# Chunk 0's inverse with one operand in PSUM and GpSimd beside it, block-diagonal inverses in its solves, and chunk 1's grams ahead of them

## What is computed

```python
y[t]  = q[t] @ state
v_old = state.T @ k_n[t]
state = state + beta[t] * outer(k_n[t], v[t] - v_old)
```

## Time and profile before

| | |
|---|---|
| median of three runs | 999.22 us |
| the profiled execution's own time | 1000.15 us |
| its span in the profile | 998.2 us |
| TensorE's granted clock, mean over the span | 0.993 of 2.4 GHz |
| busy time: TensorE, VectorE, ScalarE, GpSimd | 981.7, 583.1, 419.2, 25.4 us |

### The profile page before, as it was taken

The page is one execution under the profiler, slowest core; times in us unless marked ns, Lnnn a source line. Parts: engine busy times, 40 slices in busy tenths (PEclk is TensorE's granted clock), DMA queues, the critical chain, the costliest instruction groups (busy, mean ns, idle before and its releaser), DMA issues.

```text
span 998.2 us, 24906 instructions
## 1 busy us (share of the span) xinstructions
PE 981.7 (98%) x10566; PEld 804.3 (81%) x10566; DVE 583.1 (58%) x1465; ACT 419.2 (42%) x749; POOL 25.4 (3%) x34
## 2 busy tenths in 40 slices
PE   6899999999999999999999999999999999999998
PEld 6578788888888888888888888888888888888887
DVE  7769878776877687769535774433434334334332
ACT  4777544433434434424445553333333233333332
POOL 2510000000000000000000000000000000000000
PEclk9889999999999999999999999999999999999999
DMA  6342232003200410020003411001010010000000
GB/s 217 97 160 72 69 97 77 10 18 94 76 10 18 114 56 18 18 65 33 2 12 128 158 64 64 1 1 64 0 64 1 1 64 1 27 6 1 32 1 32
DMA packets 28413, 50.97 MB, mean 51 GB/s; under 512 B 2320, under 2 KB 15760, under 8 KB 28304
## 3 DMA queue, kind: packets, MB, share of 16 engines
q1 hardware_dynamic: 28304, 49.39, 15.3%
HBM read 39.94 MB, written 9.44 MB: 49 GB/s over the span
## 4 chain that ended last, share of the span: by engine, by line
PE 96%; ACT 2%; issue 1%; DMA 1%; DVE 0%; SPq 0%; DVEq 0%; ACTq 0%
PE psum L1120 40%; PE psum L1096 39%; PE psum L903 3%; PE psum L880 2%; PE psum L972 2%; PE psum L920 2%; PE psum L856 1%; PE psum L1009 1%; PE psum L929 1%; PE psum L1017 1%; PE psum L1040 1%; PE psum L1004 1%; ACT ring L622 1%; PE psum L1013 0%; DMA kt_sb<-in_k_t 0%
## 5 line engine op out<-in xcount | busy, mean ns | idle before, releaser
L1120 PE MATMUL psum<-g_hi,w 128*128 128x512 f32 x1152 | 392.1, 395 | 0.1
L1096 PE MATMUL psum<-x_hi,w 128*128 128x512 f32 x1152 | 387.0, 390 | 0.0
L1382 DVE TENSOR_TENSOR g_lo<-act_g,g_hi 128x512 fp32r<-128x512 f32 x192 | 132.6, 691 | 214.5 <-ACT g_hi L746 214.3
L1120 PEld LDWEIGHTS psum<-g_hi,w 128*128 128x128 f32 x1152 | 216.1, 188 | 50.8 <-issue 2.0
L1096 PEld LDWEIGHTS psum<-x_hi,w 128*128 128x128 f32 x1152 | 216.2, 188 | 45.6 <-issue 0.2
L746 ACT ACTIVATE g_hi<-act_g 128x512 fp32r<-128x512 f32 x192 | 121.4, 632 | 273.3 <-PE psum L1120 239.4
L1120 PE MATMUL psum<-g_lo,w 128*128 128x512 f32 x576 | 224.6, 390 | 0.0
L1096 PE MATMUL psum<-x_lo,w 128*128 128x512 f32 x576 | 224.1, 389 | 0.0
L1376 DVE TENSOR_TENSOR act_g<-act_g 128x512 f32<-128x512 f32 x96 | 66.4, 692 | 112.9 <-ACT act_g L739 112.9
L1096 PEld LDWEIGHTS psum<-x_lo,w 128*128 128x128 f32 x576 | 108.1, 188 | 22.4 <-issue 0.2
L1120 PEld LDWEIGHTS psum<-g_lo,w 128*128 128x128 f32 x576 | 108.2, 188 | 20.6
(11 more groups left out here) (101 smaller groups left out, 607.5 us busy)
## 6 DMA issues: line engine op xcount, KB each, us to landing
kt_sb<-in_k_t SPq DMA_DIRECT2D x24, 256.0 KB, 4.0
qt_sb<-in_q_t SPq DMA_DIRECT2D x24, 256.0 KB, 3.6
kn_sb<-in_k_n SPq DMA_DIRECT2D x20, 256.0 KB, 4.1
ring<-in_v_s SPq DMA_DIRECT2D x24, 192.0 KB, 2.7
between_layers<-y_out SPq DMA_DIRECT2D x6, 768.0 KB, 5.1
x_sb<-between_layers SPq DMA_DIRECT2D x6, 768.0 KB, 5.7
result<-y_out SPq DMA_DIRECT2D x5, 768.0 KB, 3.9
wi_st<-in_w_in SPq DMA_DIRECT2D x7, 384.0 KB, 3.1
```

Source lines behind the costliest of these rows:

```text
L1096: ins = pe.matmul(h_ps[n % 2][:, :], w_in_part(layer, f // GW, part)[:, kt, fs], x[:, kt, :], start=(kt == 0 and j == 0), stop=(kt == KT - ...
L1120: ins = pe.matmul(acc[kt][:, :], w_out_part(layer, f // GW, part)[:, f % GW, ds], g[n % 2][:, :], start=(f == 0 and j == 0), stop=(f == NF ...
L1382: dve.tensor_tensor(g_lo[n % 2][:, :], act_g[n % 2][:, :], g_hi[n % 2][:, :].bitcast(F32), ALU.subtract).then_inc(g_lo_ready, 1)
```

## The change

It does the following.

1. VectorE's inverse of chunk 0 writes the scaled diagonal blocks into PSUM banks 0 and 1 (`diag_ps`) and the products of each step into bank 2, so that each of its instructions has at most one input in SBUF. `x_inv` stays in SBUF. The later chunks' inverses are as they were.
2. GpSimd no longer waits for `xc`. It clears a new tile `xc_bd`, scales the values of chunk 0 (four instructions, in place of ScalarE's 32), takes the low parts of groups 0 and 1, and masks; after `xc` it copies the inverses of blocks k = 1 to 3 into `xc_bd`, 12 copies, as block-diagonal 128x128 matrices, and then takes the low parts of groups 2 and 3 (group 3 was VectorE's).
3. `first_solve` for k = 1 to 3 uses one 128x128 matmul for a head where there were four of 32x32.
4. The grams of chunk 1, all four, are made before chunk 0's solves and go to a tile of their own, `gram1`. `gram1` and `xc_bd` lie where the weights of the last two groups come later, so ScalarE waits for `s_done` before it writes group 7.
5. Order: TensorE's `keep_busy` instructions start at j = 25, use bank 3, and are longer between the stages; ScalarE cuts groups 2 and 3 before the solves; SyncE issues group 2 ahead of group 3; VectorE starts chunk 1's inverse and does its first three steps before `x_low_first`.

```diff
+        xc_bd = ahead_of_last.enter_context(nc.sbuf_tensor("xc_bd", [P, (NB - 1) * H, P], F32))
+        gram1 = [ahead_of_last.enter_context(nc.sbuf_tensor(f"gram1_{b}", [P, H, LATE], F32)) for b in range(B)]
...
         def g_ps(m):
             if m < B:
                 return bank[2 * m], bank[2 * m + 1]
-            return (bank[6], bank[7]) if m == B else (bank[5], bank[7])
+            if m < 2 * B:
+                return kq_ps(m - B)
+            return bank[5], bank[7]
 
         def kq_ps(m):
             if m < B:
-                return ((bank[2], bank[3]), (bank[4], bank[5]), (bank[6], bank[7]))[m % (B - 1)]
+                return ((bank[6], bank[7]), (bank[4], bank[5]))[m % 2]
...
         def gd_ps(n, hp):
-            return bank[hp] if n == 1 else bank[(5, 7)[hp]]
+            return bank[3 + hp] if n == 1 else bank[(5, 7)[hp]]
+
+        diag_ps = psum[:, 0:2, :].rearrange("p k c -> p (k c)").rearrange("p (r j) -> p r j", j=BLK)
+        spare_ps = bank[3]
...
-        FIRST_PIECES = (0, 2, 4, 6, 8, 10, 12, 13, 15, 16, 18, 19, 21, 23, 25, 27, 29, BLK - 1)
         EARLY = 3
+        BY_POOL = EARLY + 1
+        AHEAD = 3
+        FIRST_PIECES = (AHEAD, 5, 7, 9, 11, 12, 14, 15, 17, 18, 20, 21, 23, 25, 26, 28, 29, BLK - 1)
...
-            at = ({0: 1, 1: 2, 2: 3}, {4: 1, 5: 2, 6: 3}, {5: 2, 6: 3})[min(t, 2)]
-            ahead = {11: 0, 12: 1} if t else {12: 0}
+            at = ({}, {4: 1, 5: 2, 6: 3}, {5: 2, 6: 3})[min(t, 2)]
...
-            load_weights(0, EARLY, w_in1, w_out1)
             load_weights(0, 2, w_in1, w_out1)
+            load_weights(0, EARLY, w_in1, w_out1)
...
+            def scaled_first(k):
+
+                pool.wait_ge(v_loaded[k], 16)
+                pool.wait_ge(norm_turned, 1)
+                values = ring[:, k, :, :].rearrange("p (a h) e -> p a h e", h=2)
+                by = norm_t[:, 0, k * H:(k + 1) * H].rearrange("p (h a) -> p a h", h=2).unsqueeze(3).to_broadcast([P, HP, 2, D])
+                pool.tensor_tensor(values, values, by, ALU.mult).then_inc(scaled0, 1)
+
+            def block_diagonal(k):
+
+                pool.wait_ge(bd_zero, 1)
+                for b in range(B):
+                    wait(pool, bd_ready, (k - 1) * B + b)
+                    pool.tensor_copy(xc_bd[block_rows(b), (k - 1) * H:k * H, block_rows(b)],
+                                     xc[block_rows(b), k * H:(k + 1) * H, :]).then_inc(bd_ready, 1)
...
-            pool.wait_ge(xc_ready, 1)
+            pool.memset(xc_bd[:, :, :], 0.0).then_inc(bd_zero, 1)
+            scaled_first(0)
             low_parts(0)
+            low_parts(1)
+            for k in range(1, NB):
+                scaled_first(k)
             for m in range(B):
...
-            low_parts(1)
+            pool.wait_ge(xc_ready, 1)
+            pool.wait_ge(kq_ready, 2 * B)
+            for k in range(1, NB):
+                block_diagonal(k)
+            pool.wait_ge(bd_ready, B * (NB - 1))
             pool.memset(x_inv[:, :, :], 0.0).then_inc(x_zero, 1)
             low_parts(2)
+            low_parts(3)
...
+                if not layer and g == NG - 1:
+                    act.wait_ge(s_done, B * NB)
...
-            gd_out(1, 0)
-            gd_out(1, 1)
-            for m in range(B):
-                kq_out(m)
             split_weights(0, 0, 0)
             split_weights(0, 0, 1)
             split_weights(0, 1, 0)
+            gd_out(1, 0)
+            gd_out(1, 1)
             split_weights(0, 1, 1)
-            for k in range(NB):
-                scaled_first(k, 0, H)
+            for m in range(B):
+                kq_out(m)
+            for m in range(B, 2 * B):
+                gram_out(m)
+            split_weights(0, 2, 0)
+            split_weights(0, 2, 1)
+            split_weights(0, EARLY, 0)
+            split_weights(0, EARLY, 1)
...
+                    if k:
+                        ins = pe.matmul(chain_ps[part][:, at:at + D], xc_bd[:, place(k - 1, j), :], ring[:, k, j, :],
+                                        start=True, stop=True)
+                        continue
...
+            for m in range(B, 2 * B):
+                gram_of(m)
             pe.wait_ge(mask_ready, 2)
-            for j in range(19, BLK - 1):
+            for j in range(25, BLK - 1):
                 pe.wait_ge(inv_chain, inv_count(j))
-                keep_busy(2 * P, bank[0])
+                keep_busy(2 * P, spare_ps)
...
             for k in range(1, NB):
-                keep_busy(2 * P, bank[0])
-                for part in range(HALVES):
-                    first_substitute(k, part)
+                keep_busy(3 * P, spare_ps)
+                first_substitute(k, 0)
+                keep_busy(P, spare_ps)
+                first_substitute(k, 1)
                 for part in range(HALVES):
                     first_solve(k, part)
...
-            gram_of(B)
             keep_busy(4 * P, bank[1])
+            keep_busy(P, bank[1])
...
-                dve.tensor_tensor(diag[:, :, :], diag[:, :, :], ngain[:, :].unsqueeze(1).to_broadcast(every),
+                if n == 0:
+                    dve.wait_ge(gram_ready, 4)
+                dve.tensor_tensor(scaled_diag(n), diag[:, :, :], ngain[:, :].unsqueeze(1).to_broadcast(every),
                                   ALU.mult).then_inc(inv_chain, 1)
...
+                    products = tmp[:, :] if n else bank[2]
...
             gains_value(1)
             gains_turn(1)
+            start_inverse(1)
+            inverse_steps(1, 0, AHEAD)
             for m in range(B):
                 x_low_first(m)
-            start_inverse(1)
```

More of the change, by code:

```diff
@@ L94, in delta_rule_then_two_moe @@
         first_layer = ExitStack()
-        weights = [[first_layer.enter_context(nc.sbuf_tensor(f"w1_{g}", [P, 2, 2, GW * DM], F32R)) for g in range(NG)]]
+        weights = [[first_layer.enter_context(nc.sbuf_tensor(f"w1_{g}", [P, 2, 2, GW * DM], F32R)) for g in range(NG - 2)]]
+        ahead_of_last = ExitStack()
+        xc_bd = ahead_of_last.enter_context(nc.sbuf_tensor("xc_bd", [P, (NB - 1) * H, P], F32))
+        gram1 = [ahead_of_last.enter_context(nc.sbuf_tensor(f"gram1_{b}", [P, H, LATE], F32)) for b in range(B)]
+        ahead_of_last.close()
+        weights[0] += [first_layer.enter_context(nc.sbuf_tensor(f"w1_{g}", [P, 2, 2, GW * DM], F32R)) for g in range(NG - 2, NG)]
         att = ExitStack()
@@ L614, in gain_root @@
                 act.activation(droot[:, :], squares(), ACT.Sqrt, bias=tiny[:, 0:1]).then_inc(droot_ready, 1)
-            def scaled_first(k, first, past):
-                act.wait_ge(v_loaded[k], 16)
-                act.wait_ge(norm_turned, 1)
-                for j in range(first, past):
-                    at = place(k, j)
-                    act.activation(ring[:, k, j, :], ring[:, k, j, :], ACT.Copy, scale=norm_t[:, 0, at:at + 1]).then_inc(scaled0, 1)
             def kq_out(m):
@@ L646, in gram_out @@
                 act.wait_ge(gram_done, m + 1)
-                if m >= B:
+                if m >= 2 * B:
                     act.wait_ge(first_s_done, HALVES * (NB - 1))
-                    wait(act, s_done, B * NB * (m // B - 1))
+                if m >= 3 * B:
+                    act.wait_ge(s_done, B * NB * (m // B - 1))
                 for hp in range(2):
                     blocks = g_ps(m)[hp][0:LATE, 0:HP * LATE].rearrange("p (h t) -> p h t", h=HP)
-                    act.activation(gram[m % B][0:LATE, hp * HP:(hp + 1) * HP, :], blocks, ACT.Copy).then_inc(gram_ready, 1)
+                    act.activation(gram_at_chunk(m // B)[m % B][0:LATE, hp * HP:(hp + 1) * HP, :], blocks, ACT.Copy).then_inc(gram_ready, 1)
             def solved(k, b):
@@ L1243, in inverse_steps @@
                         rows = rows[0:1]
-                    outer = [tmp[:, begin:begin + count * w].rearrange("p (r c) -> p r c", r=count) for _, count, begin in rows]
+                    products = tmp[:, :] if n else bank[2]
+                    outer = [products[:, begin:begin + count * w].rearrange("p (r c) -> p r c", r=count) for _, count, begin in rows]
                     for odd, count, _ in rows:
@@ L1247, in inverse_steps @@
                         chain(n, at - 1 + odd if j > 1 else at)
-                        dve.tensor_tensor(outer[odd], diag[:, j:j + 1, j + 1:BLK].to_broadcast(part),
+                        dve.tensor_tensor(outer[odd], scaled_diag(n)[:, j:j + 1, j + 1:BLK].to_broadcast(part),
                                           x_inv[:, odd:j + 1:2, j:j + 1].to_broadcast(part), ALU.mult).then_inc(inv_chain, 1)
```

80 lines of the change are left out of this document (43 added, 37 removed).

## The result

The changed kernel takes 1006.14 us (median of 4 runs, 1006.04 to 1006.44), the kernel before beside it 999.6: a ratio of 1.0066, 95% interval 1.0048 to 1.0083. That is slower, outside the predicted range. Its profiled execution took 1006.44 us, with a span of 1004.7 [before: 1000.15 and 998.2].

What follows compares the result with a forecast made beforehand. TensorE, busy 98% of the span, was taken as the bound, apart from the start before the first product. Terms -3.6 - 1.8 (outputs at full clock) - 2.6 = -8.0 us from 1000.15 gave 992.15, forecast 991.2; range 988.5 to 998.8.

Steps and rivals of the forecast that it cites:

- The inverse in PSUM: Chunk 0's inverse on VectorE, 122 instructions writing PSUM: 0 us, from -1.2 to +14.
- ScalarE freed: ScalarE's 32 scalings leave, so its first copy of u_sb comes earlier: 1.1 us on the chain.
- The rivals of expensive PSUM writes and of no overlap: Chunk 0's inverse: PSUM writes not overlapped, inverse 34.9 us, net +6.5, 1005.7 us; chance 0.09.
- GpSimd blocking VectorE in spite of PSUM: Chunk 0's inverse: GpSimd's reads would add up to 16 us; chance 0.02, counted with the slower case.
- Twice the columns, twice that: 67 ns.: Block-diagonal solve, 128-column weights: 67 ns a row, 0.54 us a half; bounds 33 and 188 ns.
- The stages at full clock.: Chunk 0's solves after T (xc ready, 37.2): 3.25 us a stage, outputs at T + 12.75 instead of T + 16.4, -3.6 us.
- the rival: TensorE's clock falls all the same, at T + 5 (T: xc ready, 37.2): 998 us, chance 0.14; later or partly 994.5, 0.18.
- the 1.1 of the issue stall, which followed the 1.5 MB load at 40.9 that has moved.: Second-block solve: the 1.09 us issue stall goes, counted within the -3.6 us before the outputs.
- Three grams of 0.85 us ... -2.6.: Steps 0 to 2: three grams leave TensorE's list, where nothing is idle, -2.6 us.
- the 1.08 us ... comes from `turn_inverse` and stays: Before chunk 1's first solve: the 1.08 us there comes from turn_inverse and stays.
- Chunk 1's grams ... fit between 28 and 33.7.: Ahead of xc: chunk 1's grams and their copies, 0.9 us an item, fit there; cover 0.9 us.
- The 12 copies: 0.: GpSimd's copies into xc_bd: 0 us, at most 0.6 each, ready before the solves with least margin 0.9 us.

Runs made afterwards that it cites:

- e4: The changed kernel with the scaled diagonal blocks and products of chunk 0's inverse in SBUF again, GpSimd still beside it: 1019.0 us, ratio 1.0197.
- e2: The changed kernel with the kn_sb loads for items 2 and 3 issued ahead of weight group 4's load: 1002.09 us, ratio 1.0031.
- e5: e3 with chunk 1's grams back in steps 0 to 2 and keep_busy again from j = 19: 999.06 us, ratio 0.9996.
- e8: e3 with one keep_busy of 2P between the stages in place of 3P and P: 1000.03 us, ratio 1.0001.
- e9: e3 without the 12 copies into xc_bd and without its memset: 996.32 us, ratio 0.9969.
- e11: e9 with chunk 1's grams where the kernel before has them: 996.86 us, ratio 0.9974.
- e3: The changed kernel with both the old 32x32 solves and two kn_sb loads ahead of group 4's weights: 997.79 us, ratio 0.9982.
- e6: e3 with fewer busy instructions ahead of the first solve (from j = 29, and 4P in place of 4P and 3P): 997.65 us, ratio 0.9986.
- e10: e9 with the fewer busy instructions of e6: 995.64 us, ratio 0.9967.
- e1: The changed kernel with chunk 0's solves of blocks 1 to 3 as 32x32 matmuls again, copies into xc_bd still made: 999.31 us, ratio 1.0001.
- e7: The changed kernel, 128x128 solves kept, with one keep_busy of 2P between the stages in place of 3P and P: 1002.02 us, ratio 1.0033.

## Why the prediction was wrong

**Right.** The inverse in PSUM at 0 us (it gave -0.2 from a range of -1.2 to +14), GpSimd beside it at 0, and ScalarE freed (first copy of `u_sb` at 37.73, before 39.08). The rule of the Trainium skill (VectorE: DVE Perf Modes, The TRN2 errata), from which I had estimated 65 ns more an instruction and a sum of about 0, is not borne out: 251 and 240 ns against 246. That measured the output in PSUM too, of which no row of before had anything. The rivals of expensive PSUM writes and of no overlap are gone, and that of GpSimd blocking VectorE in spite of PSUM too (the same 251 and 240 ns, with GpSimd at work; e4 shows what the blocking is). The copies into `xc_bd` released no solve late in the profile, the wait for `s_done` cost nothing, and `x_lo` was not late because of `start_inverse`.

**"Twice the columns, twice that: 67 ns."** This step failed first. Sixteen rows take 1.96 us at full clock, 122 ns each, and 3.65 at half, 228 ns. The bounds held (33 and 188 at full clock), the choice between them did not. The single loads, by tile (shortest, median, longest in ns), first those of e2 at full clock, then those of the changed kernel's 64-column rows:

```profile
L1003 PEld LDWEIGHTS psum<-ring,xc_bd x48: 186/192/192, 44.1 to 53.8; 128*128 128x128 f32 x48
```

```profile
L1086 PEld LDWEIGHTS psum<-u_sb,kn_sb x32: 132/138/138, 70.5 to 71.4; 128*64 128x64 f32 x32
```

A load of 64 columns more takes 54 ns more, yet a row takes 89 more (122 against 33). A row of 33 ns is shorter than its own 64 columns take to load at that rate, so these rows must load beside one another; two such weights fit into 128 columns, and one of 128 leaves no room. That last reason is argued, not tested. The Trainium skill (TensorE: Matmul & The Clock Gate, LDWEIGHTS) states a load time of the columns divided by 1.2, in ns: the 54 agree with its 53 for the 64 columns more, while the recorded loads themselves (192 and 138 ns) are each 85 ns above it. An estimate by it for 128 columns is 107 ns, nearer to the 122 measured than my 67. By 122 ns a stage would have cost 0.88 us more than I charged (16 x 0.055), 2.6 over three, and the range's upper end would have moved with it.

**"The stages at full clock."** The clock fell at 43.2 us, that is at T + 6 where the rival had T + 5. I had given this 0.14, and 0.18 to a part of it, because `keep_busy` and the larger solves fill the stages. They did fill them (TensorE busy 4.28 of 5.00 us from 40 to 45, all of the next 5) and the clock stayed at 0.50; so the argument "the fall came behind a stretch with a third of it idle" was no ground. The outputs then ran at half clock for most of their length: 7.26 us from their start to the first product, where I had 4.85. The rival's price, 998, was too low for the same reason as the forecast: it took 0.54 us a half for a solve, 1.07 at half clock, and one at half clock is 3.6 for both halves. With that in the rival's sum (1.5 us more in each of two stages at half clock, 0.9 in the one at full) it stands at 1002; with the load's 3.8 below, at 1005.7, and 1006.1 was measured. It comes this close partly because two small errors cancel: the start was another 0.8 us longer (0.4 before the outputs, 0.6 behind, 0.2 back from an earlier `xc`), and the grams gave more than 2.6.

**"the 1.1 of the issue stall, which followed the 1.5 MB load at 40.9 that has moved."** It did not go with the load. 0.71 us of such a stall stand at 40.38 in the changed kernel with the DMA engines at 0.02 from 40 to 45 us, and e5, e8, e9 and e11 have stalls of 0.40 to 0.67 us in their first solves. So the load was not its cause, or not its only one; what is stays open.

**"Three grams of 0.85 us ... -2.6."** The mechanism was right: in e3 the second state change comes 3.3 us earlier behind the first product (11.75 against 15.05), and 2.4 of them reach the end. That it is 3.3 and not 2.6 has two small reasons. The nine rows of a product take longer behind a gram than behind another product, as the chain of the kernel before shows (start, length, what), twice 0.2 us:

```profile
63.72 2.26 PE psum L1096 x9
...
73.30 2.04 PE psum L1096 x9
```

And the first product is recorded 0.3 us early there, beside `keep_busy` (0.79 us long, 0.47 in the changed kernel). What I left out is the load. These are, in the kernel before, the rows that need `kn_sb`, the issues on SyncE's queue, and the times from issue to landing of `kn_sb`:

```profile
75.27 1.14 PE L1040 MATMUL psum<-u_sb,kn_sb 128*64 128x48 f32 x32
```

```profile
68.38 0.38 SPq L454 DMA_DIRECT2D y_out<-in_w_in  x1
68.80 0.49 SPq L456 DMA_DIRECT2D y_out<-in_w_out  x1
69.34 7.45 SPq L427 DMA_DIRECT2D kn_sb<-in_k_n  x4
```

```profile
DMA to landing us min/median/max: 3.3/4.3/5.3
```

`kn_sb` was issued from 69.34 on and needed at 75.27, with up to 5.3 us to landing, so it was there with as little as 0.6 us to spare. Group 4's load (`y_out`) already stood in front of it. In the changed kernel it no longer waits for VectorE, and `kn_sb` is issued 5.9 us behind the first product instead of 9.1; but it now takes 7.98 us to land, in a denser row of loads. Counted from the first product it comes at most 0.5 us earlier (13.9 us behind it, before 14.4 at the latest), while TensorE asks for it 3.3 us earlier (11.8 and 15.05). I had named group 4's load as one that "no longer waits", and asked only when its own data are needed, not when those behind it are. It cost 2.16 + 0.61 + 1.05 us, of which 1.66 are not the wait but the clock behind it. Then "the 1.08 us ... comes from `turn_inverse` and stays" is wrong too: when TensorE comes earlier it grows to 1.63 to 2.17 (e2, e3, e6, e8, e9, e10; 1.08 to 1.11 in the others), because VectorE's chain for chunk 1 now binds. In e3 that is 0.8 of the 3.3 us.

**"Chunk 1's grams ... fit between 28 and 33.7."** On ScalarE they did. TensorE's own list I did not add up: at half clock it starts the first solve 0.75 to 4.0 us behind `xc` (e6 0.75, e1 2.4, e3 3.0, e2 4.0), against 0.1 in the changed kernel, where the clock was full. So this cost the changed kernel nothing in its profile.

**"The 12 copies: 0."** True for the wait that I looked at, and so true in the changed kernel, where the solves are later still. With the 32x32 solves they push two low parts onto VectorE's gains; without them the medians are 1.5 to 2.2 us lower (three pairs). I had the rule on two SBUF inputs in hand for the inverse and did not ask it again for the instructions that GpSimd would meet next.

**Open.** Why TensorE's clock falls in one execution and not in another. In e1, e2, e6, e8 and e10 it is at half from 21 to 24 us with TensorE recorded as busy without a gap; in the changed kernel, e7 and e9 it is at full there. In the changed kernel and e7 it falls at about 43, in e2 (larger solves, same filler) it doesn't. e3's record shows 1.00 where its durations (5.56 us for the 64 rows of the grams, as in e1 at 0.50) say half, so the clock column isn't always to be trusted. No edit here controls it. So a part of the loss stays open: the form of the solves costs 3.3 us at full clock, but why the changed kernel's solves also lost the clock, and those of e1 and e2 did not, no run here shows.

## What to carry to other kernels

Ask what an instruction's form loads, not only what it computes: replacing four 32x32 matmuls by one of 128x128 with zeros in it saved three quarters of the instructions and doubled the time (0.88 to 1.96 us). When work is taken out of a stretch that the bottleneck fills, list what lands or ends just before the points that move forward (a load, the other engine's chain), with its margin now; what has under 1 us of margin takes the gain back. Where the engine's own list is the critical path, price filler as work: here it cost 2.4 us and the clock fell all the same. When the same kernel can run in either clock, read a gain off one profile only after a look at the clock in both.

## What was not expected of the hardware

- A matmul of fp32 with 128x128 weights and 48 columns moving: 122 ns a row at 2.4 GHz and 228 at 1.2; the 32x32 form 14 and 23 (0.88 and 1.50 us for 64 rows).
- VectorE with both inputs in SBUF beside GpSimd can wait for the whole of GpSimd's instruction: 0.25 us becomes 1.87, 0.19 becomes 1.73, while GpSimd's 1.80 stay 1.80. With at most one input in SBUF this is gone at no cost (251 and 240 ns against 246).
- The granted clock stood at 0.50 for 10 us with TensorE recorded as busy all the time (45 to 55 us in the changed kernel). It also fell behind waits of 2.16 (changed kernel), 2.17 (e2) and 2.04 us (e8), and not behind 1.84 (e3) and 1.91 (e9). But the length of the last wait alone doesn't decide it: at the outputs it fell behind 0.78 us (e2) and 1.23 (e1, e3), and not behind 0.97 (e9) and 1.24 (e6). The two waits whose cost behind them could be read cost about their own length again (1.66 behind 2.16, about 2 behind 2.17).
